# Attention two units at a time in one pair of banks, with q and k loaded apart from v, in a fused attention and two-layer kernel

## The chip, the cores and the metric

The kernel runs on one core of one Trainium2 chip. The metric is the device time of one execution in microseconds (us). Lower is better.

## The reference, cut to what matters

Attention is computed inside chunks of 64 tokens (8 batches, 8 heads, 9 chunks each, head size 64); its output, 4608 tokens by 512, goes through two layers of the same shape, the first with a leaky activation, the second with `h - tanh(h)`.

```python
scores = scale * np.matmul(q_c, k_c.transpose(0, 1, 2, 4, 3))     # per chunk and head, 64 x 64
scores = scores - np.max(scores, axis=-1, keepdims=True)
attn = np.exp(scores)
attn = attn / (np.sum(attn, axis=-1, keepdims=True) + 1e-09)
out = np.matmul(attn, v_c)
...
h = x @ w_in                      # 4608 x 512 @ 512 x 2048
g = np.maximum(h, 0.0) + alpha * np.minimum(h, 0.0)      # layer 1;  layer 2: g = h - np.tanh(h)
return g @ w_out                  # 4608 x 2048 @ 2048 x 512
```

## The kernel before, in words

The tokens are cut into six superblocks of 768. A run `s` is one superblock of one layer: runs 0 to 5 are layer 1, runs 6 to 11 are layer 2. Each run has a phase A (the product with `w_in`, as seven products of a Strassen scheme for each of eight pairs of slices; every operand is split into a high and a low part in a reduced format, so that one fp32 product is three matmuls, L561 to L563) and a phase B (the product with `w_out`, L590 to L592 in layer 1).

Phase B of layer 1 has 32 steps `n`. In each, TensorE (PE) does one unit of `w_out`, 12 matmuls of 128x384. ScalarE (ACT) makes the high part of the operand two units ahead (`high_g`, L811), VectorE (DVE) its low part (`low_g`, L1068). There are three slots, so `high_g(n + 2)` waits until unit n - 1 is done, and PE waits at unit n for the low part of it. The weights come through a ring of four buffers of 1 MB, filled by SyncE's queue (SP); one buffer lasts four steps.

The attention of the next superblock is threaded through phase B of runs 0 to 4. A superblock has six attention units (`UPS` is 6) of two chunks. `UNIT_STEPS` says at which step each begins, and what happens in step n follows from the unit's age, n minus that step. The pieces of a unit are:

- `scores` on PE: 32 small matmul records of 64x64 (16 instructions), line L477;
- `shift` on DVE: the row maximum (L941) and its subtraction (L945), reading the bank in PSUM;
- `exponent` on ACT (L738);
- `normalize` on DVE: row sum (L954), plus epsilon (L956), reciprocal (L958), scaling (L960);
- `transpose_attn` on PE: four transposes (L484); `place_attnT` on ACT copies the result to SBUF;
- `output` on PE: 32 records again (L497); `copy_x` on ACT takes the result to `x_raw`.

Before, scores and shift are at age 0, normalize at age 1, the transposes at age 3, the output at age 4. In every engine's program the attention pieces of step n stand ahead of that step's other work: on PE ahead of the unit's 12 matmuls, on DVE ahead of `low_g(n + 2)`. Each unit has a pair of PSUM banks for itself: scores, then the transposes, then the outputs in the same place.

After step 19 the operands of the next run are made from `x_raw`: `high_x` on ACT, `x_sum_of` (L985) and `low_x` (L989) on DVE, in bundles of one to three a step, the last at step 31. At step 16 both DVE and ACT read two finished sums out of the banks (`read_y`, L1080 on DVE), and again after step 31.

The weight preparation runs on GpSimd (POOL) from run 0 into run 3. `qkv` holds two units; a unit is loaded by two DMAs of 384 KB (L1220), which wait on `pv_done`, the outputs of the unit that used the buffer.

Of the kernel before, what the change touches and what calls it, by code (L numbers as in the profile page):

```python
# [39 lines left out]
UNIT_STEPS = (1, 5, 9, 14, 17, 21)  # L40
# [89 lines left out]
def fused_kernel(nc, chunks, weights, alpha, out):  # L130
# [6 lines left out]
    with ctx:  # L137
# [25 lines left out]
        attnT = sb("attnT", [P, G * UNIT, P])  # L163
# [10 lines left out]
        more_s4 = attnT[:, :, :].rearrange("x b n -> x (b n)").rearrange("x (i n) -> x i n", i=2)  # L174
# [9 lines left out]
        qkv_in = [sem(f"qkv_in{i}") for i in range(2)]  # L184
# [86 lines left out]
        def banks_of(u):  # L271

            if opening(u):
                pair = (0, 2, 1, 3, 0, 2)[u]
                return banks[:, 2 * pair - 2:2 * pair, :] if pair else a_bank
            return {1: banks[:, 4:6, :], 4: banks[:, 0:2, :]}.get(u % UPS, a_bank)

        def attnT_of(u):
            return attnT_first[:, u % 2, :, :] if opening(u) else attnT[:, :, :]
# [68 lines left out]
        def unit_age(s, u, n):  # L348

            return n - UNIT_STEPS[u] if s < SUPER - 1 else -1  # L350

# [94 lines left out]
        def _(pe):  # L446
# [8 lines left out]
            def scores(u):  # L455
# [4 lines left out]
                else:  # L460
                    s = u // UPS - 1
                    pe.wait_ge(qkv_in[u % 2], (u // 2 - UPS // 2 + 1) * UNIT * 16)
                    pe.wait_ge(x_copied, u if u % UPS in (0, 3) else u - 1)
                    if u % UPS == 1:
                        pe.wait_ge(c12_ready, after_pairs(s, PAIRS - 1))
                        pe.wait_ge(c21_ready, after_pairs(s, PAIRS - 1))
                    elif u % UPS == 4:
                        pe.wait_ge(y_even_read, y_reads(s, 2))
                        pe.wait_ge(y_odd_read, y_reads(s, 2))
                bank, q, k = banks_of(u), qkv_of(u, 0), qkv_of(u, 1)  # L470
# [10 lines left out]
            def transpose_attn(u):  # L481
                pe.wait_ge(attn_ready, u + 1)
                for b in range(G * UNIT):
                    last = nc.tensor.transpose(banks_of(u)[:, 0, b * P:(b + 1) * P],  # L484
# [3 lines left out]
            def output(u):  # L488
                pe.wait_ge(attnT_ready, u + 1)
                bank, v, attn = banks_of(u), qkv_of(u, 2), attnT_of(u)  # L490
# [11 lines left out]
            def bank_free(s, i, p):  # L502
# [5 lines left out]
                elif layer_of(s - 1) == 0:  # L508
                    if i == 1:
                        if s < SUPER:  # L510
                            pe.wait_ge(x_copied, UPS * s + 5)
# [54 lines left out]
            def second_product(s, n, halves=(0, 1)):  # L566
# [4 lines left out]
                for i in halves:  # L571
# [5 lines left out]
                    for t in range(2):  # L577
                        if f == 0:
# [4 lines left out]
                            elif m == 2:  # L583
                                if s < SUPER - 1:
                                    pe.wait_ge(x_copied, UPS * (s + 1) + 2)
# [44 lines left out]
            def attention(s, n):  # L630
                for u in range(UPS):
# [79 lines left out]
        def _(act):  # L711
# [28 lines left out]
            def place_attnT(u):  # L740
                act.wait_ge(attnT_done, u + 1)
                if not opening(u):
                    act.wait_ge(pv_done, u)
# [4 lines left out]
                nc.scalar.copy(attnT_of(u).rearrange("x b n -> x (b n)"), banks_of(u)[:, 0, :]).then_inc(attnT_ready, 1)  # L748

            def copy_x(u):  # L750
                act.wait_ge(pv_done, u + 1)
                if u and u % UPS == 0:
                    act.wait_ge(xlo_ready, OPERANDS * (u // UPS))
                nc.scalar.copy(x_columns(u), banks_of(u)[:, :, 0:G * P].rearrange("x r (g n) -> x r g n", g=G)).then_inc(x_copied, 1)
# [75 lines left out]
            def attention(s, n):  # L830
                for u in range(UPS):
                    age = unit_age(s, u, n)
                    if age == 0:
                        exponent(UPS * (s + 1) + u)
                    elif age == 3:
                        place_attnT(UPS * (s + 1) + u)
                    elif age == 4:
# [20 lines left out]
            def phase_b(s):  # L858
                layer = layer_of(s)
                for n in range(units_in(layer)):  # L860
# [5 lines left out]
                    if n == 1:  # L866
# [4 lines left out]
                    if s < SUPER - 1:  # L871
                        if n == 19:
                            high_x(s + 1, B11)
                            high_x(s + 1, B21)
                        elif n == 27:
                            high_x(s + 1, T1)
                        elif n == 28:
                            high_x(s + 1, T2)
                            high_x(s + 1, T3)
                        elif n == 29:  # L880
                            high_x(s + 1, B22)
                            high_x(s + 1, T4)
# [52 lines left out]
        def _(dve):  # L935
            def shift(u):
                dve.wait_ge(scores_done, u + 1)
                if u:
                    dve.wait_ge(shifted, u)
                heads = banks_of(u)[:, :, 0:G * P].rearrange("x r (b j) -> x r b j", j=CHUNK)  # L940
# [149 lines left out]
            def attention(s, n):  # L1090
                for u in range(UPS):
                    age = unit_age(s, u, n)
                    if age == 0:
# [274 lines left out]
```

## Time and profile before

| | us |
|---|---|
| median of 3 runs (lowest, highest) | 1601.37 (1599.87, 1602.28) |
| the profiled execution | 1604.22 |
| its span, first to last instruction | 1602.4 |
| PE busy (share of the span) | 1572.0 (98%) |
| DVE busy | 996.5 (62%) |
| ACT busy | 620.4 (39%) |
| POOL busy | 326.3 (20%) |

The busy time of an engine is the union of its instructions. Matmuls are pipelined and overlap in these records, so for PE the distance from one start to the next is the better measure than busy time; that is what the prediction reads.

### The profile page before, as it was taken

To read this page: it belongs to the slowest core of one execution; us is meant where nothing else is said; L and a number is where in the kernel's file an instruction comes from. 1 tells how busy PE (TensorE), PEld (TensorE's weight loads), DVE (VectorE), ACT (ScalarE), POOL (GpSimd) and SP (SyncE) were. 2 spreads that over 40 slices of the span, in tenths; PEclk is the share of its full clock that TensorE was granted. 3 is DMA by queue.
4 is the path that set the end of the run, shared out by engine and by line. 5 is a ranking of instruction groups with operands and counts; after the bars stand their busy time and mean duration, and the time that the engine had idled before them with its cause. 6 is when DMAs were issued, how large, how long until landed. Compare 5 with 4: busy or idle time off the path is not lost.

```text
span 1602.4 us, 26552 instructions
## 1 busy us (share of the span) xinstructions
PE 1572.0 (98%) x10512; PEld 1480.7 (92%) x10512; DVE 996.5 (62%) x1371; ACT 620.4 (39%) x947; POOL 326.3 (20%) x434
## 2 busy tenths in 40 slices
PE   5999999999999999999999999999999999999999
PEld 4999999999999999999999989989988988988987
DVE  6987678858767775766764643653652662562542
ACT  4566334524534553453452331331331331241221
POOL 6673557656564200000000000000000000000000
PEclk8999999999999999999999999999999999999999
DMA  7585997698889648647646736735845844844851
GB/s 267 215 321 198 324 369 256 224 337 315 289 293 374 217 153 298 220 165 264 223 144 241 264 133 220 279 134 219 294 142 194 303 147 171 315 158 147 288 181 68
DMA packets 72938, 375.04 MB, mean 234 GB/s; under 512 B 9072, under 2 KB 13168, under 8 KB 38256
## 3 DMA queue, kind: packets, MB, share of 16 engines
q1 hardware_dynamic: 63216, 341.87, 59.4%
q0 software_dynamic: 9600, 31.46, 5.3%
q8 instruction: 86, 1.41, 0.4%
q14 instruction: 36, 0.29, 0.1%
HBM read 308.29 MB, written 65.01 MB: 233 GB/s over the span
## 4 chain that ended last, share of the span: by engine, by line
PE 91%; DVE 5%; DMA 2%; issue 1%; ACT 1%; POOL 0%; SPq 0%; ACTq 0%; DVEq 0%
PE banks L561 14%; PE banks L563 14%; PE banks L562 14%; PE banks L590 8%; PE banks L592 7%; PE banks L591 7%; PE banks L624 5%; PE banks L625 5%; PE banks L623 5%; PE a_bank L624 3%; PE a_bank L625 3%; PE a_bank L623 3%; DVE go_lo L1068 1%; DMA ring<-w_split 1%; PE a_bank L497 1%
## 5 line engine op out<-in xcount | busy, mean ns | idle before, releaser
L561 PE MATMUL banks<-xo_hi,ring 128*128 128x384 f32 x1344 | 451.0, 336 | 5.2 <-issue 2.4
L562 PE MATMUL banks<-xo_lo,ring 128*128 128x384 f32 x1344 | 450.1, 335 | 0.0
L563 PE MATMUL banks<-xo_hi,ring 128*128 128x384 f32 x1344 | 450.0, 335 | 0.0
L1068 DVE TENSOR_TENSOR go_lo<-g_full,go_hi 128x768 fp32r<-128x768 f32 x288 | 292.0, 1018 | 237.9 <-ACT go_hi L811 237.3
L811 ACT CAST go_hi<-g_full 128x768 fp32r<-128x768 f32 x288 | 239.7, 837 | 378.2 <-PE banks L625 223.5
L590 PE MATMUL banks<-go_hi,ring 128*128 128x384 f32 x768 | 264.4, 344 | 2.9 <-DVE go_lo L1068 2.5
L561 PEld LDWEIGHTS banks<-xo_hi,ring 128*128 128x128 f32 x1344 | 252.9, 188 | 8.1 <-issue 5.2
L592 PE MATMUL banks<-go_hi,ring 128*128 128x384 f32 x768 | 257.0, 335 | 0.0
L591 PE MATMUL banks<-go_lo,ring 128*128 128x384 f32 x768 | 256.8, 334 | 0.0
L562 PEld LDWEIGHTS banks<-xo_lo,ring 128*128 128x128 f32 x1344 | 253.0, 188 | 0.4
L563 PEld LDWEIGHTS banks<-xo_hi,ring 128*128 128x128 f32 x1344 | 253.0, 188 | 0.0
L590 PEld LDWEIGHTS banks<-go_hi,ring 128*128 128x128 f32 x768 | 144.1, 188 | 8.3 <-issue 3.0
L625 PE MATMUL banks<-ring,go_lo 128*128 128x512 f32 x384 | 149.6, 390 | 0.0
L624 PE MATMUL banks<-ring,go_hi 128*128 128x512 f32 x384 | 149.6, 390 | 0.0
L623 PE MATMUL banks<-ring,go_hi 128*128 128x512 f32 x384 | 149.4, 389 | 0.0
L591 PEld LDWEIGHTS banks<-go_lo,ring 128*128 128x128 f32 x768 | 144.3, 188 | 0.0
L592 PEld LDWEIGHTS banks<-go_hi,ring 128*128 128x128 f32 x768 | 144.1, 188 | 0.0
L1029 DVE TENSOR_TENSOR u<-s,banks 128x384 f32<-128x384 f32 x96 | 53.1, 553 | 127.5 <-PE banks L563 127.5
L771 ACT COPY s<-banks 128x384 f32<-128x384 f32 x96 | 46.3, 482 | 209.7 <-PE banks L563 209.6
L1059 DVE SCALAR_TENSOR_TENSOR g_full<-stage,alpha_rest,g_full 128x768 f32<-128x768 f32 x96 | 104.8, 1132 | 0.0
L1042 DVE TENSOR_TENSOR g_full<-u,banks 128x384 f32<-128x384 f32 x96 | 53.0, 552 | 82.1 <-PE banks L563 82.1
L800 ACT ACTIVATE stage<-g_full 128x1152 f32<-128x1152 f32 x48 | 56.1, 1169 | 121.1 <-DVE g_full L1042 121.1
(130 smaller groups left out, 1874.8 us busy)
## 6 DMA issues: line engine op xcount, KB each, us to landing
ring<-w_split SPq DMA_DIRECT2D x242, 1024.0 KB, 5.5
qkv<-in_chunks SPq DMA_DIRECT2D x60, 384.0 KB, 5.1
w_split<-ring SPq DMA_DIRECT2D x22, 1024.0 KB, 4.9
w_split<-made_first POOLq DMA_DIRECT2D x44, 256.0 KB, 5.8
w_split<-sums POOLq DMA_DIRECT2D x44, 256.0 KB, 6.0
y_between<-stage SPq DMA_DIRECT2D x12, 768.0 KB, 7.4
x_raw<-y_between SPq DMA_DIRECT2D x6, 1536.0 KB, 9.0
out<-x_raw SPq DMA_DIRECT2D x36, 256.0 KB, 6.5
```

The lines of the kernel that those rows point to most:

```text
L561: nc.tensor.matmul(h, hi, xo_hi[:, o, k, :], start=fresh and k == 0, stop=False, skip_group_check=not fresh)
L562: nc.tensor.matmul(h, hi, xo_lo[:, o, k, :], start=False, stop=False, skip_group_check=not fresh)
L563: last = nc.tensor.matmul(h, lo, xo_hi[:, o, k, :], start=False, stop=k == 1, skip_group_check=not fresh)
L590: nc.tensor.matmul(y, hi, go_hi[:, slot, t, :], start=f == 0, stop=False)
L591: nc.tensor.matmul(y, hi, go_lo[:, slot, t, :], start=False, stop=False)
L592: last = nc.tensor.matmul(y, lo, go_hi[:, slot, t, :], start=False, stop=last_unit)
L623: nc.tensor.matmul(y, hi, w_hi, start=n == 0, stop=False)
L624: nc.tensor.matmul(y, hi, w_lo, start=False, stop=False)
L625: last = nc.tensor.matmul(y, lo, w_hi, start=False, stop=n == 15)
L811: nc.scalar.copy(go_hi[:, go_slot(s, n), :, :], g_of(n)).then_inc(ghi_ready, 1)
L1059: nc.vector.scalar_tensor_tensor(mine, part[:, p % 2, 2 * half:2 * half + 2, :], alpha_rest[:, f:f + 1], mine, ALU.mult, ALU.add).then_inc ...
L1068: nc.vector.tensor_tensor(go_lo[:, slot, :, :], g_of(n), go_hi[:, slot, :, :], ALU.subtract).then_inc(glo_ready, 1)
```

## The change

Units are taken in pairs. `UNIT_STEPS` becomes (1, 7, 13), the step of each pair; both units' scores are at age 0, the shifts at ages 0 and 1, the normalizations at ages 2 and 3, both units' transposes at age 4, both outputs at age 6. The two units of a pair share one pair of banks: scores and outputs of the even unit in columns 0 to 255 of both banks, of the odd one in columns 256 to 511; the transposes of the even unit in the first bank, of the odd one in the second. So a transpose overwrites scores of both units and waits for both (`together(u)`). The middle pair of units is in banks 4 and 5, the first and the last in `a_bank`. `attnT` gets a second buffer.

```diff
-UNIT_STEPS = (1, 5, 9, 14, 17, 21)
+UNIT_STEPS = (1, 7, 13)
...
+            return banks[:, 4:6, :] if u % UPS // 2 == 1 else a_bank
+        def score_bank(u):
+            at = 0 if opening(u) else u % 2 * G * P
+            return banks_of(u)[:, :, at:at + G * P]
+        def transposed_bank(u):
+            return banks_of(u)[:, 0 if opening(u) else u % 2, :]
+        def together(u):
+            return u + 1 if opening(u) else u + 2 - u % 2
...
             def transpose_attn(u):
-                pe.wait_ge(attn_ready, u + 1)
+                pe.wait_ge(attn_ready, together(u))
...
             def output(u):
-                pe.wait_ge(attnT_ready, u + 1)
+                pe.wait_ge(attnT_ready, together(u))
+                if not opening(u):
+                    pe.wait_ge(v_in[u % 2], (u // 2 - UPS // 2 + 1) * UNIT * 16)
...
             def shift(u):
-                dve.wait_ge(scores_done, u + 1)
+                dve.wait_ge(scores_done, together(u))
```

The ages on PE, ACT and DVE, and the operations for the next run's operands, one a step:

```diff
                     if age == 0:
                         scores(UPS * (s + 1) + u)
-                    elif age == 3:
+                    elif age == 4:
                         transpose_attn(UPS * (s + 1) + u)
-                    elif age == 4:
+                    elif age == 6:
                         output(UPS * (s + 1) + u)
...
-                    if age == 0:
+                    if age == u % 2:
                         shift(UPS * (s + 1) + u)
-                    elif age == 1:
+                    elif age == u % 2 + 2:
                         normalize(UPS * (s + 1) + u)
...
-                    if n == 3:
+                    if n == (6 if layer == 0 else 3):
                         activate(s, PAIRS - 1)
...
+                        if n in (17, 18):
+                            low_x(s + 1, B11 if n == 17 else B21)
+                        elif 21 <= n < 25:
+                            x_sum_of(s + 1, (T1, T2, T3, T4)[n - 21])
+                        elif 0 <= n - 25 < OPERANDS - 2:
+                            low_x(s + 1, n - 23)
```

(before: `low_x` at 20 and 23, `x_sum_of` one at 26, two at 27, one at 28, `low_x` at 28, 29, twice at 30, and at 31).

The loads: q and k of a unit (two DMAs of 256 KB) now wait on `scores_done`, v (two of 128 KB) on `pv_done`. They stand at four places of the queue in place of six.

```diff
+            def load_ahead(s, stage):
+                first = UPS * s
+                if stage == 0:
+                    for u in (first, first + 1):
+                        load_qk(u)
+                        load_v(u)
+                elif stage == 1:
+                    load_qk(first + 2)
+                    load_qk(first + 3)
+                elif stage == 2:
+                    load_v(first + 2)
+                    load_v(first + 3)
+                    load_qk(first + 4)
+                    load_qk(first + 5)
+                elif stage == 3:
+                    load_v(first + 4)
+                    load_v(first + 5)
...
-                    if s < SUPER - 1 and q in (8, 9, 15, 16, 17, 18):
-                        load_unit(UPS * (s + 1) + (8, 9, 15, 16, 17, 18).index(q))
+                    if s < SUPER - 1 and q in (8, 15, 16, 18):
+                        load_ahead(s + 1, (8, 15, 16, 18).index(q))
```

Three places of the instruction order show it. On DVE, from step 1 of phase B of run 4, before (L941 and L945 are `shift`, L954 to L960 `normalize`, L1068 `low_g`, L1059 `activate`):

```order
L941 TENSOR_REDUCE row_max<-a_bank 128x8 [waits shifted,scores_done]
L945 TENSOR_TENSOR probs<-a_bank,row_max 128x2x4x64 [waits attnT_done,max_ready]
L1068 TENSOR_TENSOR go_lo<-g_full,go_hi 128x768 [waits ghi_ready]
L954 TENSOR_REDUCE row_sum<-probs 128x8 [waits attn_ready,exp_done]
L956 TENSOR_SCALAR row_sum<-row_sum 128x8 [waits norm_step]
L958 RECIPROCAL row_inv<-row_sum 128x8 [waits norm_step]
L960 TENSOR_TENSOR probs<-probs,row_inv 128x512 [waits norm_step]
L1068 TENSOR_TENSOR go_lo<-g_full,go_hi 128x768 [waits ghi_ready]
L1059 SCALAR_TENSOR_TENSOR g_full<-stage,alpha_rest,g_full 128x768 [waits c11_read,part_ready]
L1059 SCALAR_TENSOR_TENSOR g_full<-stage,alpha_rest,g_full 128x768
```

The same place of the changed kernel, whose lines are a few numbers higher (L944 and L948 `shift`, L957 to L963 `normalize`, L1071 `low_g`):

```order
L944 TENSOR_REDUCE row_max<-a_bank 128x8 [waits shifted,scores_done]
L948 TENSOR_TENSOR probs<-a_bank,row_max 128x2x4x64 [waits attnT_done,max_ready]
L1071 TENSOR_TENSOR go_lo<-g_full,go_hi 128x768 [waits ghi_ready]
L944 TENSOR_REDUCE row_max<-a_bank 128x8 [waits shifted,scores_done]
L948 TENSOR_TENSOR probs<-a_bank,row_max 128x2x4x64 [waits attnT_done,max_ready]
L1071 TENSOR_TENSOR go_lo<-g_full,go_hi 128x768 [waits ghi_ready]
L957 TENSOR_REDUCE row_sum<-probs 128x8 [waits attn_ready,exp_done]
L959 TENSOR_SCALAR row_sum<-row_sum 128x8 [waits norm_step]
L961 RECIPROCAL row_inv<-row_sum 128x8 [waits norm_step]
L963 TENSOR_TENSOR probs<-probs,row_inv 128x512 [waits norm_step]
L1071 TENSOR_TENSOR go_lo<-g_full,go_hi 128x768 [waits ghi_ready]
L957 TENSOR_REDUCE row_sum<-probs 128x8 [waits attn_ready,exp_done]
```

The second shift and the second normalization now stand between the first shift and the end of the pair's preparation, with a `low_g` between any two of them.

On PE, step 5 of phase B of run 1 before, where the output of one unit and the scores of the next meet (L590 to L592 are the unit of weights):

```order
L592 MATMUL banks<-go_hi,ring 128x384
L497 MATMUL a_bank<-attnT,qkv 64x64 [waits attnT_ready]
L497 MATMUL a_bank<-attnT,qkv 64x64 x15
L477 MATMUL banks<-qkv 64x64 [waits c12_ready,c21_ready,x_copied,qkv_in1]
L477 MATMUL banks<-qkv 64x64 x15
L590 MATMUL banks<-go_hi,ring 128x384 [waits glo_ready,ring_in1]
```

Step 7 of the same phase in the changed kernel (L509 output, L487 scores, L600 to L602 the unit of weights):

```order
L602 MATMUL banks<-go_hi,ring 128x384
L509 MATMUL a_bank<-attnT,qkv 64x64 [waits v_in0,attnT_ready]
L509 MATMUL a_bank<-attnT,qkv 64x64 x15
L509 MATMUL a_bank<-attnT,qkv 64x64 [waits v_in1,attnT_ready]
L509 MATMUL a_bank<-attnT,qkv 64x64 x15
L487 MATMUL banks<-qkv 64x64 [waits c21_ready,c12_ready,qk_in0]
L487 MATMUL banks<-qkv 64x64 x15
L487 MATMUL banks<-qkv 64x64 [waits c21_ready,c12_ready,qk_in1]
L487 MATMUL banks<-qkv 64x64 x15
L600 MATMUL banks<-go_hi,ring 128x384 [waits glo_ready,ring_in1]
```

Four batches of small matmuls now stand in a row where there were two.

On SP, in phase B of run 4 before, from the load of a ring buffer (L1255) and of the third unit on:

```order
L1255 DMA ring<-w_split 128x2048 [waits block_done] x6
L1220 DMA qkv<-in_chunks 128x768 [waits pv_done]
L1220 DMA qkv<-in_chunks 128x768
L1255 DMA ring<-w_split 128x2048 [waits block_done]
L1220 DMA qkv<-in_chunks 128x768 [waits pv_done]
L1220 DMA qkv<-in_chunks 128x768
```

The same place of the changed kernel (L1274 ring, L1211 q and k, L1220 v):

```order
L1274 DMA ring<-w_split 128x2048 [waits block_done] x7
L1211 DMA qkv<-in_chunks 128x512 [waits scores_done]
L1211 DMA qkv<-in_chunks 128x512
L1211 DMA qkv<-in_chunks 128x512 [waits scores_done]
L1211 DMA qkv<-in_chunks 128x512
L1274 DMA ring<-w_split 128x2048 [waits block_done]
L1220 DMA qkv<-in_chunks 128x256 [waits pv_done]
L1220 DMA qkv<-in_chunks 128x256
```

q and k of two units follow one ring buffer at once, where a whole unit followed it, and v comes one ring buffer later.

## Rows read from the trace of the kernel before

**Rows 1.** Timeline of PE, run 4, phase B: start, duration, instruction, count.

```profile
665.41 0.34 PE L592 MATMUL banks<-go_hi,ring 128*128 128x384 f32 x1
...
667.05 0.34 PE L591 MATMUL banks<-go_lo,ring 128*128 128x384 f32 x1
...
672.95 0.34 PE L592 MATMUL banks<-go_hi,ring 128*128 128x384 f32 x1
...
673.74 0.34 PE L591 MATMUL banks<-go_lo,ring 128*128 128x384 f32 x1
...
685.54 0.34 PE L592 MATMUL banks<-go_hi,ring 128*128 128x384 f32 x1
...
686.72 0.34 PE L591 MATMUL banks<-go_lo,ring 128*128 128x384 f32 x1
```

**Rows 2.** Timeline of PE, run 0: the late transposes and the unit behind them.

```profile
107.77 0.66 PE L484 MATMUL a_bank<-ident,probs 128*128 128x128 f32 x4 [0.82 <-DVE probs L960]
109.27 0.41 PE L590 MATMUL banks<-go_hi,ring 128*128 128x384 f32 x1 [0.85 <-DVE go_lo L1068]
```

**Rows 3.** Timeline of PE: step 16 in run 2; first and last of five late gaps.

```profile
182.50 0.41 PE L561 MATMUL banks<-xo_hi,ring 128*128 128x384 f32 x1 [0.92 <-issue]
...
420.25 0.34 PE L592 MATMUL banks<-go_hi,ring 128*128 128x384 f32 x1
...
420.98 0.34 PE L591 MATMUL banks<-go_lo,ring 128*128 128x384 f32 x1
...
462.27 0.41 PE L561 MATMUL banks<-xo_hi,ring 128*128 128x384 f32 x1 [0.62 <-issue]
```

**Rows 4.** Timeline of DVE ahead of the first of those gaps.

```profile
175.86 5.60 DVE L989 TENSOR_TENSOR xo_lo<-x_raw,xo_hi 128x768 fp32r<-128x768 f32 x4
```

**Rows 5.** Timeline of DVE, run 4, one attention unit from its scores on.

```profile
666.91 0.69 DVE L941 TENSOR_REDUCE row_max<-banks 128x8 f32<-128x512 f32 x1 [1.56 <-PE banks L477]
...
668.24 0.95 DVE L1068 TENSOR_TENSOR go_lo<-g_full,go_hi 128x768 fp32r<-128x768 f32 x1
669.11 0.68 DVE L954 TENSOR_REDUCE row_sum<-probs 128x8 f32<-128x512 f32 x1
...
670.26 0.69 DVE L960 TENSOR_TENSOR probs<-probs,row_inv 128x512 f32<-128x512 f32 x1
670.87 0.95 DVE L1068 TENSOR_TENSOR go_lo<-g_full,go_hi 128x768 fp32r<-128x768 f32 x1
...
694.32 1.01 DVE L1080 COPY stage<-banks 128x384 f32<-128x384 f32 x2
```

**Rows 6.** DVE's L1068 alone in three phases B: stretch, length, busy (count), clock, DMA.

```profile
99.00:165.00 66.00, 27.86 (x26) 1.00 0.66 239
...
381.00:444.00 63.00, 28.23 (x25) 1.00 0.81 270
...
656.00:719.00 63.00, 23.74 (x25) 1.00 0.52 180
```

**Rows 7.** Timeline of DVE, runs 0 and 1: the first unit of the phase.

```profile
105.36 0.69 DVE L954 TENSOR_REDUCE row_sum<-probs 128x8 f32<-128x512 f32 x1 [1.39 <-ACT probs L738]
...
241.73 0.68 DVE L941 TENSOR_REDUCE row_max<-a_bank 128x8 f32<-128x512 f32 x1
```

**Rows 8.** Timeline of PE, run 1, behind the scores of the first unit.

```profile
240.81 0.34 PE L591 MATMUL banks<-go_lo,ring 128*128 128x384 f32 x1
```

**Rows 9.** PE in run 2 behind a ring load; a ring load's issue and its landing.

```profile
374.32 0.44 PE L561 MATMUL banks<-xo_hi,ring 128*128 128x384 f32 x1 [1.18 <-DMA ring<-w_split]
...
L1255 SPq DMA_DIRECT2D ring<-w_split x1: 327/327/327, 356.5 to 356.5; - x1
...
DMA to landing us min/median/max: 11.6/11.6/11.6
```

**Rows 10.** Timeline of PE in the opening, and its granted clock (fourth number) there.

```profile
28.10 1.13 PE L497 MATMUL banks<-stage,g_full 64*64 64x64 f32 x32 [3.32 <-ACT stage L748]
...
35.00:40.00 5.00, 4.61 (x14) 0.50 0.99 390
```

More of the change, by code:

```diff
@@ L183, in fused_kernel @@
         ring_in = [sem(f"ring_in{i}") for i in range(RING)]
-        qkv_in = [sem(f"qkv_in{i}") for i in range(2)]
+        qk_in, v_in = [sem(f"qk_in{i}") for i in range(2)], [sem(f"v_in{i}") for i in range(2)]
         qkv_first_in = [sem(f"qkv_first_in{i}") for i in range(UPS)]
@@ L1210, in load_unit, with load_qk, load_v @@
             def load_unit(u):
-                if opening(u):
-                    dst, landed = qkv_first[:, u, :], qkv_first_in[u]
-                else:
-                    dst, landed = qkv[:, u % 2, :], qkv_in[u % 2]
-                    if u < UPS + 2:
-                        sp.wait_ge(wlo_ready, raw_use(PAIRS - 1) + 1)
-                    else:
-                        sp.wait_ge(pv_done, u - 1)
-                for i in range(UNIT):
-                    sp.dma_start(dst[:, i * 3 * G * P:(i + 1) * 3 * G * P], chunks[u * UNIT + i, :, :]).then_inc(landed, 16)
+                for i in range(UNIT):
+                    sp.dma_start(qkv_first[:, u, i * 3 * G * P:(i + 1) * 3 * G * P], chunks[u * UNIT + i, :, :]).then_inc(qkv_first_in[u], 16)
+            def load_qk(u):
+                if u < UPS + 2:
+                    sp.wait_ge(wlo_ready, raw_use(PAIRS - 1) + 1)
+                else:
+                    sp.wait_ge(scores_done, u - 1)
+                for i in range(UNIT):
+                    at = i * 3 * G * P
+                    sp.dma_start(qkv[:, u % 2, at:at + 2 * G * P], chunks[u * UNIT + i, :, 0:2 * G * P]).then_inc(qk_in[u % 2], 16)
+            def load_v(u):
+                if u < UPS + 2:
+                    sp.wait_ge(wlo_ready, raw_use(PAIRS - 1) + 1)
+                else:
+                    sp.wait_ge(pv_done, u - 1)
+                for i in range(UNIT):
+                    at = i * 3 * G * P + 2 * G * P
+                    sp.dma_start(qkv[:, u % 2, at:at + G * P], chunks[u * UNIT + i, :, 2 * G * P:3 * G * P]).then_inc(v_in[u % 2], 16)
+            def load_ahead(s, stage):
[15 more added lines that the diff above has]
+                    load_v(first + 5)
             def load_raw(c):
@@ L1293, in make_groups @@
                         store_group(s, j)
[L1294 to L1295 removed]
+                    if j in (54, 66, 72, 79):
+                        load_ahead(s + 1, (54, 66, 72, 79).index(j))
                 store_y(s, 0)
```

83 lines of the change are left out of this document (25 added, 58 removed).

## The prediction, on record before the changed kernel ran

> **What bounds the kernel now.** The page's first part first: PE is busy for 98% of the span, DVE for 62%. PE is the bound, so the change is worth what it adds to or takes from PE's own sequence. Next the timeline of PE, read by starts, since the records overlap. Behind the double batch in run 4 the L591 that begins at 667.05 and the L592 at 672.95 are 34 matmuls apart: 0.1735 us each, so a step of 12 is 2.08 us [rows 1]. What attention costs is what stands between two such matmuls beyond their own 2 x 0.174 (two starts lie there: the first matmul behind a switch starts late and so does the next).
>
> - One batch of 32 small records: 685.54 to 686.72 is 1.18, less 0.35: **0.83** [rows 1].
> - Two batches in a row: 665.41 to 667.05 is 1.64, less 0.35: **1.29** [rows 1]. So a batch costs 0.47 and the switch to it and back 0.36.
> - Four transposes: 672.95 to 673.74 is 0.79, less 0.35: **0.44** [rows 1].
>
> A phase B of before has five single batches (one stands behind transposes, as a sixth, and costs the same 0.83), three doubles and six groups of transposes: 6 x 0.83 + 3 x 1.29 + 6 x 0.44 = 11.5 us; five phases 57.5.
>
> Then the waits of PE. A wait that the timeline shows as w costs w + 0.25 from start to start (0.16 is the overlap of records, 0.09 the slow restart: the restarted record lasts 0.41 for 0.34 [rows 1, 3]). In run 0 the transposes and the unit behind them wait 0.82 and 0.85 [rows 2], 2.1 in all. At step 16 of runs 0 to 2 PE waits for `read_y`: 420.25 to 420.98 is 0.73, less 0.35, 0.38 [rows 3], three times 1.1; three more of 0.2 to 0.3 lie in steps 5 and 8 of runs 1 and 2. Together 4.0. Around the ends of runs 0 to 2 there are five gaps, the first 0.92 + 0.25 = 1.17, the last 0.62 + 0.25 = 0.87 [rows 3], together 4.9. Ahead of the first DVE has four `low_x` in one piece of 5.60 us, and `read_y` comes only behind them [rows 4]. All of before's excess is 57.5 + 4.0 + 4.9 = **66.4 us**.
>
> **Part by part.**
>
> *Batches on PE.* Now there are 2, 4, 4 and 2 batches at steps 1, 7, 13 and 19: 4 x 0.36 + 12 x 0.47 = 7.1. The six groups of transposes stand in twos; a group's four records are nearly all of its cost, so I take them at 6 x 0.44 = 2.6 (bound: a saved switch of up to 0.36 for each pair, 5 us in all; nearest is the transposes ahead of a batch, which cost their full 0.44). 9.7 a phase, **48.6** for five: a gain of 8.9.
>
> *Spread x operations.* One `x_sum_of` or `low_x` (0.95 to 1.1) with one `low_g` a step of 2.08, the last at step 29: `read_y` is no longer behind a bundle and the five gaps go, a gain of 4.9 (already counted, as they are not in 48.6). What hides them is DVE's slack behind step 20. `activate` at step 6 in place of 3 lies where DVE has nothing of attention.
>
> *The new wait.* A pair's transposes wait for both normalizations, four steps after the scores. DVE's queue between is shift, `low_g`, shift, `low_g`, normalize, `low_g`, normalize. Its durations by starts, undisturbed [rows 5]: shift 666.91 to 668.24, 1.33; `low_g` to 669.11, 0.87; normalize to 670.87, 1.76, and to the end of its last record (670.26 + 0.69 + 0.05 to PE) 1.89. The chain is 3 x 0.87 + 2 x 1.33 + 1.76 + 1.89 = **8.92 us** from `row_max`. `row_max` begins 0.03 behind the point where the unit's first matmul would regularly stand (667.05 - 0.174 = 666.88; a second batch moves both by 0.47). PE needs 4 x 2.08 = 8.33 for the four units. So even undisturbed the transposes are late by 8.92 + 0.03 - 8.33 = **0.62**. Before, the chain was one shift, one normalize and two `low_g` in three steps, 4.9 for 6.2: no wait.
>
> On top of it:
> - In the last pair `read_y` stands between (step 16): 1.01 less the overlap of 0.08, **0.93** [rows 5].
> - In runs 0 to 2 POOL runs beside. `low_g` takes 27.86/26 = 1.07 and 28.23/25 = 1.13 there, against 23.74/25 = 0.95 in run 4 [rows 6]: 0.15 more, three times; I take 0.10 for each of the two scalings. **0.65** a pair. Bounds: nothing, and twice that, since the disturbance is bunched.
> - DVE comes late into the phase: in run 1 `row_max` starts at 241.73 [rows 7], regular would be 240.81 - 0.17 + 0.47 + 0.03 = 241.14 [rows 8], so **0.6**. In run 0 the first row sum cannot start before 105.36 [rows 7] for want of the exponential; from there 1.76 + 0.87 + 1.89 + 0.4 is 110.3; the transposes were due at 107.77 - 0.98 and are now due 2.08 + 0.47 later, 109.3 [rows 2]: 1.0, near the ordinary 1.3, which I take.
>
> The Trainium skill says, in "SBUF — State Buffer", section "Who interferes with whom", that a DVE instruction with two SBUF inputs is held for the whole of a GpSimd instruction that reads SBUF, while a reduction or an operation from PSUM is not. By it exactly the three `low_g` and the two scalings of the chain are exposed, and with 0.15 for each the sum would be 0.75 in place of 0.65, 0.9 us more in nine pairs.
>
> Sum of stalls: runs 0 to 2, 9 x (0.62 + 0.65) + 3 x 0.93 + 0.6 = 14.8; runs 3 and 4, 6 x 0.62 + 2 x 0.93 = 5.6; restarts 15 x 0.09 = 1.4. **21.8 us.** Behind PE's wait are the pair's transposes and the unit's 12 matmuls; DVE catches up meanwhile, so nothing is carried to the next pair.
>
> *Loads.* In phase A of run 2 PE already waits for a ring load, 1.18 + 0.25 [rows 9]. A ring load has 12 blocks of 6 matmuls, 12.5 us. The load issued at 356.5 took 11.6 [rows 9] with one attention unit ahead of it; now two are ahead, 0.77 MB more, some 3 us at the rate at which that load moved (1 MB in queue for some 4 us): late by about 2.3, while the next one is then in time. Net **+0.9**, bounds 0 and 3. At step 4 q and k (1 MB) follow a ring load and are needed at step 7, 8 to 9 us later with the stall: taken as hidden.
>
> *Sum.* 48.6 + 21.8 + 0.9 - 66.4 = **+4.9 us**. The profiled execution had 1604.22 us (span 1602.4, 1.8 around it), 2.9 above the median of the runs; 1609.1 against it, **1606.3 us** against the median of 1601.37.
>
> **Rivals.**
> - *The chain runs everywhere at run 4's pace* and restarts are free. For it: rows 5 are exact to a few hundredths. Stalls are 15 x 0.62 + 5 x 0.93 = 14.0, sum 48.6 + 14.0 - 66.4 = -3.8: **1597.6**. It decides when the mean stall of a pair is under 17.8/15 = 1.2 us; I have 1.45. Against it: the `low_g` rows of runs 0 to 2. This is the one on the other side.
> - *The chain does not bind at all*: -17.8, **1583.6**. Against it is plain arithmetic on rows 5.
> - *Gain and loss cancel* within 0.2% (3.2 us, about what can be told from no change): bunched POOL operations that fall beside the chain. **1602 to 1604**.
> - *q and k come late at step 7.* They queue behind 1 MB. If a load of this size lands as late as the 11.6 of rows 9, PE waits about 2 us at step 7 in runs 1 to 3: +6, **1612**. Against it: phase B moves one ring buffer in 8.3 us, phase A one in 4.2.
> - *The clock falls.* In the opening PE stood for 3.32 us [rows 10] and the granted clock was 0.50 (the level of 1.2 GHz) until 40 us [rows 10]; at it a matmul takes twice its 0.174. If each of the five last pairs (2.2 us of wait, then transposes) brought one fall of some 8 us of matmuls, 5 x 4 = 20 us: **1626**. Against it: with two waits of 0.82 and 0.85 a step apart the clock of run 0's phase B was 1.00 [rows 2, 6]. The Trainium skill, "TensorE: Matmul & The Clock Gate", section "Why this matters for your kernels", warns of idle gaps between bursts in this way; the trace agrees for 3.3 us, and has none of 2.2.
>
> **How the numbers follow.** Forecast 0.56; run 4's pace everywhere 0.17; cancelled 0.08; late q and k 0.12; no binding 0.04; clock 0.03. The likeliest gives 1606.3, with its own range of 1602.5 to 1611 from the bounds (POOL 0 to 1.3 a pair, saved switches, loads). The range goes down to the pace of run 4 and up to late q and k: 1597 to 1613. Faster: no binding and most of run 4's pace, 0.16. Same: cancelled, the rest of it and the forecast's lower edge, 0.24. Slower: 0.60.
>
> **What would show it.** Right: PE waits on DVE's scaling ahead of the transposes fifteen times, about 0.5 in runs 3 and 4 and 1.4 for their last pair, more in runs 0 to 2; four batches in a row cost 2.2; no gap at the ends of runs 0 to 2. Wrong: transposes that begin without a wait, or a phase B of run 4 that is not longer (I expect +1.0: 9.7 + 2.8 + 0.3 against 11.5). A wait at step 7 on a DMA, or a clock under 1.00, would belong to the last two rivals.

## The result, and the profile after

| | median us | lowest, highest | executions |
|---|---|---|---|
| before | 1601.21 | 1599.87, 1602.28 | 4 |
| changed | 1616.13 | 1615.81, 1619.58 | 4 |

The changed kernel is slower: the ratio is 1.0095, with a 95% interval of 1.0083 to 1.0108. That is +14.9 us where +4.9 was forecast; the direction is right, the time lies outside the range. The profiled execution took 1619.58 us.

The page's first part, and the shares of the chain that ended last:

```profile
span 1617.8 us, 26627 instructions
PE 1571.1 (97%) x10512; PEld 1485.1 (92%) x10512; DVE 993.0 (61%) x1371; ACT 622.9 (39%) x947; POOL 320.6 (20%) x434
PE 86%; DVE 8%; issue 3%; DMA 2%; ACT 0%; SPq 0%; POOL 0%; DVEq 0%; ACTq 0%
```

PE is busy for as long as before (1571.1 us against 1572.0, though batches and transposes take 9 us less by starts) and the span is 15.4 us longer: the time went into waits, and a smaller part into matmuls that take longer. What PE waited for (total us, times, longest):

```profile
PE a_bank L494 <- DVE probs L963: 17.8, 11, 3.0
PE banks L494 <- DVE probs L963: 6.7, 6, 2.0
...
PE banks L571 <- DVE xo_lo L992: 2.1, 2, 1.7
```

L494 are the transposes, L963 is the scaling. Two of the 17 waits are those of the opening, 2.7 us; the other fifteen are 21.8 us, one ahead of every pair's transposes. The timeline of PE in run 4, which answers to [rows 1]:

```profile
679.47 0.34 PE L602 MATMUL banks<-go_hi,ring 128*128 128x384 f32 x1
680.27 1.09 PE L494 MATMUL a_bank<-ident,probs 128*128 128x128 f32 x8 [0.46 <-DVE probs L963]
681.12 0.42 PE L600 MATMUL banks<-go_hi,ring 128*128 128x384 f32 x1
681.38 0.34 PE L601 MATMUL banks<-go_lo,ring 128*128 128x384 f32 x1
...
683.14 0.33 PE L602 MATMUL banks<-go_hi,ring 128*128 128x384 f32 x1
...
713.82 1.09 PE L494 MATMUL a_bank<-ident,probs 128*128 128x128 f32 x8 [1.40 <-DVE probs L963]
```

And DVE's records of the same pair, which answer to [rows 5]:

```profile
671.35 0.69 DVE L944 TENSOR_REDUCE row_max<-a_bank 128x8 f32<-128x512 f32 x1 [0.52 <-PE a_bank L487]
...
679.52 0.69 DVE L963 TENSOR_TENSOR probs<-probs,row_inv 128x512 f32<-128x512 f32 x1
```

From `row_max` at 671.35 to the transposes at 680.27 it is 8.92 us, the sum that the prediction made out of rows of before. Run 4 behaves as forecast. Run 1 does not; the same place on PE there:

```profile
270.57 0.34 PE L602 MATMUL banks<-go_hi,ring 128*128 128x384 f32 x1
272.95 1.11 PE L494 MATMUL banks<-ident,probs 128*128 128x128 f32 x8 [2.04 <-DVE probs L963]
273.80 0.59 PE L600 MATMUL banks<-go_hi,ring 128*128 128x384 f32 x1
274.19 0.52 PE L601 MATMUL banks<-go_lo,ring 128*128 128x384 f32 x1
274.50 0.52 PE L602 MATMUL banks<-go_hi,ring 128*128 128x384 f32 x1
...
277.36 0.33 PE L602 MATMUL banks<-go_hi,ring 128*128 128x384 f32 x1
```

Two things differ: the wait is 2.04 in place of 0.46, and the matmuls behind it start 0.32 us apart in place of 0.174. From the transposes to the last of the unit's matmuls it is 4.41 us, against 2.87 in run 4. The windows show why (us, busy time of PE, PEld, DVE, ACT and POOL, then granted clock, DMA share, GB/s):

```profile
114.00:118.00 4.00, 4.00 (x19) 4.00 (x19) 3.04 (x4) 1.17 (x2) 0.00 (x0) 0.64 1.04 411
274.00:278.00 4.00, 4.00 (x16) 4.00 (x15) 0.83 (x1) 0.94 (x3) 3.46 (x6) 0.59 0.81 312
278.00:282.00 4.00, 4.00 (x140) 3.69 (x139) 1.09 (x2) 2.52 (x4) 3.24 (x6) 1.00 0.76 252
400.00:404.00 4.00, 4.00 (x18) 4.00 (x17) 3.44 (x4) 1.17 (x2) 1.36 (x3) 0.57 0.93 363
```

In runs 0, 1 and 2 TensorE works at the level of 1.2 GHz behind one wait each (3.04, 2.04 and 2.20), and then at 2.4 GHz again: in runs 1 and 2 for 10 or 11 matmuls, in run 0 for the transposes themselves (1.97 us in place of 1.09) and five matmuls. Each of these stretches costs 1.5 us. The longer waits come from DVE, whose queue in run 1 shows stretched operations ahead of them:

```profile
268.16 0.89 DVE L963 TENSOR_TENSOR probs<-probs,row_inv 128x512 f32<-128x512 f32 x1
268.97 1.15 DVE L1071 TENSOR_TENSOR go_lo<-g_full,go_hi 128x768 fp32r<-128x768 f32 x1
...
271.19 1.70 DVE L963 TENSOR_TENSOR probs<-probs,row_inv 128x512 f32<-128x512 f32 x1
```

The scaling takes 1.70 us for 0.69 in run 4. Measured by PE's starts, in the same way as before's 66.4, the excess over regular matmuls in the five phases B and the phases A between them is 68.0 us before (the 1.4 of the wait for the ring load [rows 9] included) and 82.6 after, 14.6 more.

### The profile page after: what moved, and what is told of

Same layout as the page of the kernel before. It is cut to its first block, busy times and chain, and to the rows that moved or that the text cites. A ratio compares the mean times of both kernels' runs of the same rounds, so it can differ in the third digit from the quotient of the medians.

```text
span 1617.8 us, 26627 instructions
## 1 busy us (share of the span) xinstructions
PE 1571.1 (97%) x10512; PEld 1485.1 (92%) x10512; DVE 993.0 (61%) x1371; ACT 622.9 (39%) x947; POOL 320.6 (20%) x434
## 3 DMA queue, kind: packets, MB, share of 16 engines
q8 instruction: 86, 1.41, 0.4%
## 4 chain that ended last, share of the span: by engine, by line
PE 86%; DVE 8%; issue 3%; DMA 2%; ACT 0%; SPq 0%; POOL 0%; DVEq 0%; ACTq 0%
PE banks L571 14%; PE banks L573 14%; PE banks L572 14%; PE banks L600 6%; PE banks L601 6%; PE banks L602 6%; PE banks L635 5%; PE banks L634 5%; PE banks L633 5%; PE a_bank L635 3%; PE a_bank L633 3%; PE a_bank L634 3%; DVE probs L963 2%; DVE row_sum L957 1%; DVE row_max L944 1%
## 5 line engine op out<-in xcount | busy, mean ns | idle before, releaser
L1071 DVE TENSOR_TENSOR go_lo<-g_full,go_hi 128x768 fp32r<-128x768 f32 x288 | 290.8, 1014 | 240.7 <-ACT go_hi L821 240.0
L600 PE MATMUL banks<-go_hi,ring 128*128 128x384 f32 x768 | 262.8, 342 | 0.8 <-DVE stage L1083 0.7
L602 PE MATMUL banks<-go_hi,ring 128*128 128x384 f32 x768 | 258.2, 336 | 0.0
L600 PEld LDWEIGHTS banks<-go_hi,ring 128*128 128x128 f32 x768 | 145.5, 189 | 4.0 <-DVE stage L1083 1.6
L602 PEld LDWEIGHTS banks<-go_hi,ring 128*128 128x128 f32 x768 | 145.4, 189 | 0.0
```

Of the source, the lines that this page charges most:

```text
L600: nc.tensor.matmul(y, hi, go_hi[:, slot, t, :], start=f == 0, stop=False)
L602: last = nc.tensor.matmul(y, lo, go_hi[:, slot, t, :], start=False, stop=last_unit)
L1071: nc.vector.tensor_tensor(go_lo[:, slot, :, :], g_of(n), go_hi[:, slot, :, :], ALU.subtract).then_inc(glo_ready, 1)
```

## The experiments

The theory going in was that the time is lost at one place, the late transposes, in three parts: DVE's chain is longer than four units, POOL stretches it in runs 0 to 2, and the clock falls behind the longest waits. The rivals: the new loads, the spread x operations, and a cost of the pairs themselves that a moved transpose would not give back. Line numbers in rows are each kernel's own and differ by a few from those of the changed kernel. Each ratio is against the kernel before in the same session (medians 1602.5, 1601.4 and 1602.3 us in the three sessions).

**The transposes a step later.** Nothing else moves; outputs stay at age 6.

```diff
-                    elif age == 4:
+                    elif age == 5:
                         transpose_attn(UPS * (s + 1) + u)
...
-                    elif age == 4:
+                    elif age == 5:
                         place_attnT(UPS * (s + 1) + u)
```

> One edit on the changed kernel: a pair's transposes and their copies at age 5 in place of 4 (PE and ACT), nothing else. Theory 1 (the chain of shifts, normalizations and low parts is longer than the four units PE has for it, and the clock falls come from those waits): PE has 10.4 us for a chain of 8.9 (undisturbed) to about 11.5 (last pair beside POOL), so nearly all of the 26.8 us of waits ahead of transposes and all three stretches at half clock (4.6 us) go, about 1616 - 30 = 1586 us, granted clock 1.00 in every phase B. Theory 2 (DVE has too much work in the paired steps, so the wait only moves to the low parts of the operand): PE then waits for go_lo in steps 5 to 8, and the time is above 1606 us. Theory 3 (the batches or the loads cost it): no change, 1616 us.

Measured: 1601.26 us, ratio 0.9990 (0.9980 to 1.0). So 15 us come back (17 by the ratios), as much as the change had cost. Yet the time is 15 above the expectation. What PE waited for now, loads and low parts:

```profile
PE banks L571 <- DMA ring<-w_split: 3.1, 2, 2.0
PE banks L600 <- DVE go_lo L1071: 1.9, 5, 0.8
...
PE a_bank L487 <- DMA qkv<-in_chunks: 1.2, 2, 0.9
PE banks L487 <- DMA qkv<-in_chunks: 1.2, 2, 0.8
```

The fifteen waits for the scaling are gone and so is the half clock. In their place stand waits for loads that the changed kernel does not show: 2.4 us for q and k (L487 is the scores), 3.1 for the weights' ring. By starts, PE's waiting between the attention's first and last phase is 17.5 us in the profiled execution: 4.0 for q, k and v, 3.6 for the ring, 3.9 in gaps for which the profile names nothing, and the rest for low parts, `read_y` and the ends of the runs. Ahead of the ring load that is 2.04 late, SP's queue in run 3 shows this:

```profile
487.49 0.92 SPq L1211 DMA_DIRECT2D qkv<-in_chunks  x2
488.45 2.46 SPq L1220 DMA_DIRECT2D qkv<-in_chunks  x2
490.95 1.40 SPq L1211 DMA_DIRECT2D qkv<-in_chunks  x2
492.40 1.41 SPq L1220 DMA_DIRECT2D qkv<-in_chunks  x2
493.86 30.48 SPq L1274 DMA_DIRECT2D ring<-w_split  x7
```

The eight DMAs of the first pair take 6.4 us to issue, and the next ring load stands behind them. For q and k it is plausible that the late transposes had covered late loads: they are issued behind step 4 and needed at step 7, and PE's wait at step 5 lies between. For the ring it is not shown: these waits are in phase A, where PE does not wait for attention, and the two kernels with a longer chain (last experiment), whose transposes are late, have them too (1.30 and 1.41; 0.59). The kernel before has one of 1.18 [rows 9].

**POOL held until run 2 is over.**

```diff
             pool.wait_ge(wlo_ready, BLOCKS)
+            pool.wait_ge(block_done, done(2, BLOCKS - 1))
             load_raw2(0)
```

> One edit on the changed kernel: POOL begins the preparation of the second layer's weights only after run 2 has ended, so POOL is idle in runs 1 and 2 and busy in runs 3 and 4. If POOL's instructions are what makes the waits of runs 0 to 3 longer than run 4's 0.45, 0.46 and 1.36 us, runs 1 and 2 now have waits like run 4's (about 3 us a phase with restarts, in place of 6.9 and 6.3) and no half clock, and run 4 has 5 to 7 us of them. If it is something of the early runs themselves (DVE late into the phase, a load), runs 1 and 2 keep their waits. The total is left about the same, 1612 to 1620 us.

Measured: 1617.63 us, one execution. The transposes of the first and the last pair of run 1, and of the last pair of run 3, where POOL now works:

```profile
252.81 1.09 PE L495 MATMUL a_bank<-ident,probs 128*128 128x128 f32 x8 [0.46 <-DVE probs L964]
...
286.32 0.87 PE L495 MATMUL a_bank<-ident,probs 128*128 128x128 f32 x6 [1.39 <-DVE probs L964]
...
567.10 1.09 PE L495 MATMUL a_bank<-ident,probs 128*128 128x128 f32 x8 [1.95 <-DVE probs L964]
```

Without POOL the six waits of runs 1 and 2 are 0.46, 0.46, 1.39, 0.46, 0.33 and 1.39: run 4's, to a hundredth in five of six (in the changed kernel 1.78, 2.04, 1.92, 2.20, 1.40 and 1.44), and neither run has a stretch at half clock. The waits came up in run 4 (1.25, 1.60, 1.44) instead, and a wait of 1.55 for a ring load appeared at 777 us. That POOL makes the excess in runs 1 and 2 is shown; the total says nothing, since the work only moved. Run 0 is unchanged (2.94 with half clock behind it, 1.01, 1.44), but it was not tested: POOL works there in both kernels (33.1 and 32.6 us between 95 and 165). The changed kernel's trace says what its first chain holds. From `row_max` at 102.51 to the transposes at 113.50 it is 10.99 us, 2.07 over the undisturbed 8.92: 1.0 because `low_g(4)` waits for ACT, which comes late to the first exponential after waiting 4.47 for raw weights to load, and 1.1 in the two scalings, 1.27 and 1.18 in place of 0.69.

The Trainium skill, "SBUF — State Buffer", section "Who interferes with whom", says that a DVE operation with two SBUF inputs is held while GpSimd reads SBUF and a reduction is not. The runs agree: scaling and low part are stretched with POOL beside (1.70 and 1.15) and take 0.69 and 0.95 without, and no reduction in runs 0 to 3 of the changed kernel takes more than 0.69.

**The x operations back in their old places.** On ACT `high_x` returns to n = 19, 27, 28, 29, and on DVE:

```diff
-                        if n in (17, 18):
-                            low_x(s + 1, B11 if n == 17 else B21)
-                        elif 21 <= n < 25:
-                            x_sum_of(s + 1, (T1, T2, T3, T4)[n - 21])
-                        elif 0 <= n - 25 < OPERANDS - 2:
-                            low_x(s + 1, n - 23)
+                        if n == 20:
+                            low_x(s + 1, B11)
+                        elif n == 23:
+                            low_x(s + 1, B21)
...
+                        elif n == 31:
+                            low_x(s + 1, T4)
```

> One edit on the changed kernel: the operations for the next run's operands in their old bundles (ACT and DVE), attention as changed. If spreading them removed the gaps at the ends of runs 0 to 2 (4.9 us before, 1.2 us left), the time is about 4 us longer, 1620 us, and PE waits again behind the read_y of the ends. If the gaps went because of the paired attention, which ends six steps earlier, no change: 1616 us.

Measured: 1620.53 us, ratio 1.0119 (1.0102 to 1.0137), against 1.0095 (1.0083 to 1.0108): the intervals overlap a little, so the time alone does not settle it. The trace shows the gaps at the ends of runs 0 to 2 again, 6.5 us by starts, against 1.2 in the changed kernel and 4.9 before. The largest, at the end of run 1:

```profile
327.95 0.41 PE L600 MATMUL banks<-go_hi,ring 128*128 128x384 f32 x1 [1.79 <-DVE go_lo L1078]
```

The spread operations are a gain of about 4 us and not where the time was lost.

**Both normalizations a step earlier**, on DVE, the transposes left where they are.

```diff
-                    elif age == u % 2 + 2:
+                    elif age == u % 2 + 1:
                         normalize(UPS * (s + 1) + u)
```

> One edit on the changed kernel: the normalizations at ages 1 and 2 in place of 2 and 3, transposes still at age 4. Theory 1: one low part fewer (0.87 us) lies in the chain, 8.05 us for 8.33, and read_y is no longer in it. Runs 3 and 4 lose their waits (6.8 us), runs 0 to 2 keep about 9 of 20 us, two or more of the three stretches at half clock go: 1595 to 1599 us. Theory 2 (too much DVE work in too few steps): the three steps are fuller now, so low parts come late and PE waits for them instead: 1610 us or more.

Measured: 1612.28 us, ratio 1.0064 (1.0047 to 1.0081): 13 to 17 us above the first theory, and what the second one said (1610 or more). What PE waited for:

```profile
PE banks L600 <- DVE go_lo L1071: 7.0, 10, 2.2
...
PE banks L600 <- DVE stage L1083: 4.4, 5, 1.2
...
PE banks L600 <- ACT stage L833: 1.8, 5, 0.6
```

The transposes are in time in all fifteen places, and PE waits for the low parts and at step 16 (`stage`) in their place. The odd unit's shift and the even unit's normalization now meet in one step, and `low_g` stands behind both. So it is DVE's queue that is short of time around a pair; moving the attention inside it moves the wait to the unit behind.

**The loads, with the transposes a step later.** Three kernels on top of the first experiment: q and k of the second pair one ring load earlier; v of the first pair issued later, at q = 13; and both. The edit of the third:

```diff
-            def load_ahead(s, stage):
+            def load_ahead(s, stage, late_v=False):
...
-                        load_v(u)
+                        if not late_v:
+                            load_v(u)
...
-                    if s < SUPER - 1 and q in (8, 15, 16, 18):
-                        load_ahead(s + 1, (8, 15, 16, 18).index(q))
+                    if s < SUPER - 1 and q in (8, 14, 16, 18):
+                        load_ahead(s + 1, (8, 14, 16, 18).index(q), late_v=True)
+                    if s < SUPER - 1 and q == 13:
+                        load_v(UPS * (s + 1))
+                        load_v(UPS * (s + 1) + 1)
```

The first has only the 14 in place of 15, the second only the late v (q and k of the second pair stay at 15). The first one's expectation, the second's, and that of both together:

> Transposes at age 5 as in the first experiment, and q and k of the middle pair issued one ring buffer earlier in runs 1 to 3 and the last (four steps earlier in phase B). If the waits of PE for q and k at steps 7 and 13 of runs 0 to 2 (0.87, 0.36, 0.80 and 0.36 us) came of the issue behind the ring buffer of step 4, the ones of the middle pair go: about 2 us under the first experiment. If the transfers merely take long under load, they stay.

> Transposes at age 5, and v of the first pair not issued in the middle of phase A beside its q and k but at its end (loads of run 0 unchanged). In the first experiment the eight issues in a row held SP's queue for up to 6.4 us and the ring buffer behind them came late: PE waited 2.04 us in run 3 and 1.06 in run 2. If that is the cause both go, 3 to 4 us less than the first experiment. If it was the queue of transfers by bytes, one of the two stays.

> Both of the edits on the loads together with the transposes at age 5: the two gains add up, 5 us less than the first experiment, about 1596 us, and faster than the kernel before by 0.3 to 0.4%.

| | median us | ratio | 95% |
|---|---|---|---|
| q and k earlier | 1595.26 | 0.9958 | 0.9945 to 0.9971 |
| first v apart | 1597.25 | 0.9978 | 0.9967 to 0.9989 |
| both | 1593.82 | 0.9953 | 0.9941 to 0.9966 |

Both together are faster than the kernel before by 7.6 us. Set against the first experiment by the ratios, the gains are 5, 2 and 6 us (2, 3 to 4 and 5 were expected). They did not come the way that was expected. Moving q and k took their waits at step 7 away, but PE then waits 1.34 for v in run 2; moving v only shortened the ring waits, from 1.06 and 2.04 to 0.81 and 0.55, and the first kernel, which still issues the eight DMAs in a row (487.04 to 492.86), has none in run 3. The slowest ring load of that stretch took 13.3 us to land in the first experiment and 11.5, 13.0 and 9.8 in these three, so the time of the transfers counts beside that of the issues; which decides is open. By starts in the profiled executions the kernel with both edits has 6.8 us less than the first experiment: 3.6 of ring waits and 3.1 of gaps that have no named cause, and nothing less for q, k and v. The waits of PE in that kernel:

```profile
PE a_bank L509 <- DMA qkv<-in_chunks: 2.0, 2, 1.8
PE banks L600 <- DVE go_lo L1071: 1.5, 4, 0.8
...
PE banks L600 <- DVE stage L1083: 1.0, 2, 0.8
```

The ring waits are gone, and of the loads only v of run 2's last pair is late by more than 0.3 (L509 is the output); that wait of 1.82 has a stretch at half clock behind it. The transposes in run 4 follow a matmul with no wait:

```profile
675.01 0.34 PE L602 MATMUL banks<-go_hi,ring 128*128 128x384 f32 x1
675.19 1.03 PE L494 MATMUL banks<-ident,probs 128*128 128x128 f32 x8
675.98 0.42 PE L600 MATMUL banks<-go_hi,ring 128*128 128x384 f32 x1
```

**The same loads alone**, the transposes at age 4 as in the changed kernel.

> Both edits on the loads in the changed kernel as it was, transposes at age 4. Its profile shows no wait for q and k or a ring buffer in phases that follow a late transpose, so the waits ahead of the transposes hide late loads: no change against the changed kernel, 1616 us, within 2. If the loads cost it something of their own, 1611 us.

Measured: 1614.29 us, ratio 1.0076 (1.0064 to 1.0088), some 2 to 3 us below the changed kernel, between the two cases of the expectation. With the transposes late the loads are worth 3 us by the ratios, with the transposes in time 6 (0.9990 to 0.9953; 7.4 by the medians of two sessions). That fits one bound between the two edits, where whatever is later hides the other, but the two gains differ by less than their intervals together, so it is not shown by the times.

**A longer chain**, to ask of the clock what length of wait it takes. In runs 3 and 4 additional row sums, whose results nobody reads, stand ahead of the odd unit's own: 1, 3 and 0 in the three pairs of a run in the first kernel, 2, 4 and 1 in the second. All outputs are computed as before.

```diff
+                for _ in range((1, 3, 0)[u % UPS // 2] if u >= 4 * UPS and u % 2 else 0):
+                    nc.vector.tensor_reduce(spare[:, next(turn), :], mine, AXIS_X, ALU.add)
                 nc.vector.tensor_reduce(row_sum[:, :], mine, AXIS_X, ALU.add).then_inc(norm_step, 1)
```

> The changed kernel with more row sums (0.71 us each, results unused) ahead of the odd unit's normalization in runs 3 and 4: one for the first pair, three for the second, none for the last. If the chain on DVE sets the begin of the transposes, every added row sum adds its 0.71 us to PE's wait: 1.17 and 2.6 us in place of 0.46 and 0.47 in run 4, the last pair's 1.40 as it was. If waits of more than about 1.9 us bring the clock down, the second pair of run 4 has some ten matmuls at 0.32 us behind it and costs 1.5 us more, the first none. Sum 2 x (0.71 + 2.13) + 2 x 1.5 = +8.7 us, 1625 us. If the falls of the clock are not tied to the waits: no stretch at half clock in runs 3 and 4, +5.7 us.

> The same with two, four and one more row sums: waits of 1.88, 3.3 and 2.1 us in run 4. If waits of more than about 1.9 us bring the clock down, the second and the last pair of runs 3 and 4 have a stretch at half clock behind them and the first may or may not. Sum 2 x (1.42 + 2.84 + 0.71) + 4 x 1.5 = +16 us, 1632 us; without falls +10 us, 1626 us.

Measured: 1618.69 us, ratio 1.0104 (1.0073 to 1.0134), and 1626.57 us, ratio 1.0159 (1.0142 to 1.0176). An additional row sum takes about 0.6 us from start to start (0.71 was assumed from one that stands alone), and the waits of run 4 grow by it one for one: from 0.46, 0.47 and 1.40 to 1.06, 2.25 and 1.39, and to 1.65, 2.84 and 1.98. The totals do not test the expectation. The first lies only 2 us above the changed kernel, less than the 5.7 without any fall; in the profiled executions that is mostly run 0, whose first wait is 2.05 with no fall where it was 3.04 with one. The second agrees with the 1626 for no falls, although three fell in runs 3 and 4 (behind 3.10, 1.98 and 1.98): luck. The first kernel's pair with 2.25, and the window around it:

```profile
696.98 1.09 PE L495 MATMUL banks<-ident,probs 128*128 128x128 f32 x8 [2.25 <-DVE probs L966]
...
695.00:700.00 5.00, 3.02 (x20) 3.02 (x21) 3.56 (x7) 1.74 (x3) 0.00 (x0) 1.00 0.38 140
```

The second kernel's two last pairs:

```profile
699.97 1.09 PE L495 MATMUL banks<-ident,probs 128*128 128x128 f32 x8 [2.84 <-DVE probs L966]
...
701.08 0.34 PE L602 MATMUL banks<-go_lo,ring 128*128 128x384 f32 x1
...
717.79 1.09 PE L495 MATMUL a_bank<-ident,probs 128*128 128x128 f32 x8 [1.98 <-DVE probs L966]
...
718.90 0.52 PE L602 MATMUL banks<-go_lo,ring 128*128 128x384 f32 x1
...
717.00:722.00 5.00, 4.21 (x19) 4.21 (x20) 3.31 (x5) 1.07 (x2) 0.00 (x0) 0.69 0.47 170
```

Behind 2.84 the records keep their 0.34, behind 1.98 they take 0.52 with a granted clock of 0.69 in the window. So the theory that a wait above some length brings the clock down falls: what decides is not the length of the one wait.

## Why the prediction was wrong in size

**Right, step by step.** Two batches cost 1.29 to 1.30, four in a row 2.23, a pair's transposes 0.87 to 0.88: 9.7 a phase, as forecast; no saved switch at the transposes. The undisturbed chain is 8.92 and its lateness 0.62 (a wait of 0.46 and restart); `read_y` adds 0.93 in the last pair (1.40 against 0.47). Phase B of run 4 has an excess of 12.67, with 12.8 forecast. The gaps at the ends went down from 4.9 to 1.2. The likeliest case, waits of PE on the scaling in all fifteen places with more of it in runs 0 to 2, is what happened.

**Wrong, term by term** (the table's differences are in us against the forecast sum of +4.9):

| step | forecast | measured | difference |
|---|---|---|---|
| stalls ahead of transposes, restarts with them | 21.8 | 25.3 | +3.5 |
| `read_y` at step 16 of runs 0 to 2 | none left | 1.5 | +1.5 |
| clock | 0, a rival with 0.03 | three stretches of 1.5 | +4.6 |
| ring loads | +0.9 | -1.4 | -2.3 |
| one gap inside a batch, run 3 | none | 1.4 | +1.4 |
| gaps at the ends | none left | 1.2 | +1.2 |

4.9 + 9.9 = 14.8, against 14.6 by starts and 15.4 by the spans.

- *The POOL term was mis-sized*; of the 3.5, runs 1 and 2 hold 1.6, run 0 1.2 and run 3 0.8. "0.65 a pair" spread the mean of 0.15 for a `low_g` over the chain, and took less than that for the scalings. A mean over 25 operations is low because most of them have no POOL operation beside; in the pairs of runs 1 and 2 the waits are 1.40 to 2.20 where 0.46 and, in the last, 1.39 would stand undisturbed: 1.3, 1.6, 0.5, 1.7, 0.9 and 0.05 more, 1.0 in the mean, as the experiment with POOL held shows. The upper bound of twice 0.65 would have covered it. Run 0's first pair, "near the ordinary 1.3", was a wait of 3.04. In run 3 POOL was still at work beside the first pair (1.36), where none was reckoned.
- *`read_y` at step 16 was put at nothing on PE's side.* The three waits of 0.38 of before went into the sum as gone, with `read_y` counted only inside the chain. PE still waits there in runs 0 to 2, one unit ahead of the last pair's transposes, and it costs 0.50, 0.48 and 0.49.
- *The clock was left out of the sum.* The step that failed is "against it: with two waits of 0.82 and 0.85 a step apart the clock ... was 1.00", with the chance of 0.03 that it gave. It had rows at 0.85 and at 3.32 and none between, and its own stalls fell between; an unknown cost with a bound on each side was counted at one bound. Its price was also mis-sized: a fall lasts for some 10 matmuls and costs 1.5 us, not 4; and the falls came behind the first pairs of runs 0 and 2 and the middle pair of run 1, not behind the last pairs. The stretches vanished with the waits three times: transposes later, POOL held (runs 1 and 2), normalizations earlier (where one wait of 2.16 in run 0 is left, with no fall behind it).
- *The loads had the wrong sign.* The prediction put late ring loads on top of the stalls. In the changed kernel's profiled execution no ring load was late, and the 1.4 of before was gone. Why is open: such waits come and go between kernels whose order of loads is the same (1.06 and 2.04 in the first experiment, 1.30 and 1.41 with the longer chain, none in the changed kernel).
- *The rival of late q and k* did not occur in the changed kernel. With the transposes a step later q and k were late by 0.8 and 0.4 at step 7 of run 2, which is the rival's place, by 0.9 at step 13 of run 1 and by 0.3 in run 0.
- *A slip in the signs of being wrong:* "I expect +1.0" for run 4 does not follow from its own terms, which give 12.8 - 11.5 = 1.3. By starts it is 12.67 against 11.45, 1.2.

What stays open: which waits bring the clock down (the waits listed in the last section do not sort by length), why ring loads are late in some kernels and not in others, and the gap in run 3, for which the profile names nothing:

```profile
547.41 0.76 PE L487 MATMUL banks<-qkv 64*64 64x64 f32 x38
549.35 0.62 PE L487 MATMUL banks<-qkv 64*64 64x64 f32 x26 [1.18 <-issue]
```

It stands between two records of one batch, with all data there. It was not tried by itself. The small gaps left at the ends of the runs were not traced further either.

## What to carry to other kernels

When an edit makes the engine that bounds the kernel wait, its own delay can hide what else is late; to judge the edit's idea, take that wait away too and look at what stands behind it, here loads whose places in the queue were worth 6 us. Then check in the trace that the gain came from the wait that was aimed at; here most of it did not. Disturbance from another engine is to be taken from the rows of the place where it matters, at its worst there, and not as a mean over a stretch. Pairing and spreading were worth something in the end (7.6 us faster than before), once the transposes had one more step and the loads were split over the ring loads.

## What the runs showed of the hardware

- *Half clock behind waits of 2 us.* Behind the opening, over all traces, a stretch at the level of 1.2 GHz follows single waits of 1.82, 1.92, 1.98 (twice), 2.04, 2.20 (twice), 2.46, 2.89, 2.91, 2.94, 3.04 and 3.10, and in three cases two smaller waits in a row (such as 0.61 and 1.44, while 0.97 and 1.42 have none); none follows waits of 1.78 (twice), 1.79, 1.80, 1.92, 1.95, 2.04, 2.05, 2.09, 2.16, 2.21, 2.25, 2.45 and 2.84, and none a single wait under 1.8. Each costs about 1.5 us, with matmuls 0.32 apart for 0.174. The Trainium skill, "TensorE: Matmul & The Clock Gate", section "Why this matters for your kernels", warns of idle gaps between bursts, longer ones than these; the traces agree that falls stand behind gaps, and show them at waits of 2 us already, with full work on both sides.
- *Issues on SP.* Eight DMAs in a row took 6.4 us to issue (487.49 to 493.86), while a lone ring load's issue is 0.33 us [rows 9]. In a queue that also carries the weights that is a delay of its own; that it made a ring load late is not shown.
- *Gaps of 0.6 to 1.3 us on PE with no releaser*, in the middle of a batch or of a unit of weights (1.18 in the changed kernel; 0.95, 1.20 and 0.57 with the transposes later; 1.20 and 1.26 with POOL held), none of them in several other kernels.
